# Spreading loads over steps, weight tasks over a longer stretch, and buffers of their own, in a four-stage float32 kernel

## The reference

```python
# 8 batches, 8 heads, 576 tokens, 64 columns a head
kv  = einsum('bhsd,bhse->bhde', k, v)
out = einsum('bhsd,bhde->bhse', q, kv)
x   = out / sqrt(mean(out * out, -1) + 1e-6) * g_norm      # 4608 x 512 tokens
h   = sigmoid(x @ w_gate) * (x @ w_val)                     # 512 -> 1536
y   = h @ w_out                                             # 1536 -> 512
u   = y @ w_in                                              # 512 -> 2048
g   = u where u >= 1, 0 where u <= -1, else (u + 1)**2 / 4
out = g @ w_out2                                            # 2048 -> 512
```

## Time and profile before

| | |
|---|---|
| median of 3 runs | 1786.55 us (1785.83 to 1787.65) |
| profiled execution | 1786.39 us, span 1784.6 us |
| TensorE busy | 1689.6 us, 95% of the span |
| VectorE, ScalarE, GpSimd busy | 68%, 50%, 13% |
| mean granted TensorE clock | 0.974 |
| DMA | 278.90 MB, mean 156 GB/s |

### The profile page before, as it was taken

How to read it: one execution, slowest core, us unless ns; L and a number is a source line. 1 busy time by engine, 2 the same in 40 slices (tenths; PEclk the granted TensorE clock), 3 DMA queues, 4 the chain that set the end, 5 groups by cost and what they waited for, 6 DMA issues and landing times.

```text
span 1784.6 us, 31909 instructions
## 1 busy us (share of the span) xinstructions
PE 1689.6 (95%) x12552; PEld 1651.9 (93%) x12552; DVE 1219.7 (68%) x1723; ACT 888.7 (50%) x1611; POOL 223.5 (13%) x295
## 2 busy tenths in 40 slices
PE   8999999999899999599999889999997899999999
PEld 6789999998899999599999889999997799999999
DVE  4566766676677675477768777777774677667774
ACT  3556666555455544244445455555553444444443
POOL 6210000014443232100001320000001200000000
PEclk9999999999899999899999999999998899999999
DMA  7344434333877779553453333333337954434550
GB/s 256 125 131 138 143 129 136 107 121 117 230 212 206 199 207 276 210 167 126 134 166 138 115 125 131 132 131 132 133 133 248 299 171 136 130 120 128 147 129 36
DMA packets 229316, 278.90 MB, mean 156 GB/s; under 512 B 33072, under 2 KB 172848, under 8 KB 229168
## 3 DMA queue, kind: packets, MB, share of 16 engines
q1 hardware_dynamic: 191568, 207.66, 35.5%
q0 software_dynamic: 37600, 69.22, 13.3%
HBM read 156.76 MB, written 120.06 MB: 155 GB/s over the span
## 4 chain that ended last, share of the span: by engine, by line
PE 64%; DMA 6%; DVE 2%; issue 2%; POOL 2%; SPq 1%; ACT 1%; ACTq 0%; DVEq 0%
PE x L1496 12%; PE x L1498 12%; PE x L1497 12%; PE y L1496 6%; PE y L1498 6%; PE y L1497 6%; DMA fold_lo<-stage 3%; PE z L1496 2%; PE z L1498 2%; PE z L1497 2%; PE h L1496 1%; PE h L1498 1%; PE h L1497 1%; DMA stage<-w_in 1%; DMA g_scratch<-c_tile 1%
## 5 line engine op out<-in xcount | busy, mean ns | idle before, releaser
L1496 PE MATMUL x<-t_hi,v_lo 128*128 128x288 f32 x1664 | 502.6, 302 | 62.9 <-ACT kept L855 19.7
L1497 PE MATMUL x<-t_lo,v_hi 128*128 128x288 f32 x1664 | 496.9, 299 | 0.0
L1498 PE MATMUL x<-t_hi,v_hi 128*128 128x288 f32 x1664 | 495.8, 298 | 0.0
L1496 PEld LDWEIGHTS x<-t_hi,v_lo 128*128 128x128 f32 x1664 | 317.5, 191 | 69.9 <-ACT kept L877 20.5
L1498 PEld LDWEIGHTS x<-t_hi,v_hi 128*128 128x128 f32 x1664 | 319.0, 192 | 0.0
L1497 PEld LDWEIGHTS x<-t_lo,v_hi 128*128 128x128 f32 x1664 | 318.0, 191 | 0.2
L1496 PE MATMUL y<-t_hi,v_lo 128*128 128x288 f32 x832 | 251.5, 302 | 3.3 <-DVE c L1053 1.7
L1497 PE MATMUL y<-t_lo,v_hi 128*128 128x288 f32 x832 | 249.0, 299 | 0.0
L1498 PE MATMUL y<-t_hi,v_hi 128*128 128x288 f32 x832 | 248.2, 298 | 0.0
L1496 PE MATMUL x<-v_hi,t_lo 128*128 128x256 f32 x576 | 164.3, 285 | 6.0 <-ACT o_kept L1018 6.0
L1496 PEld LDWEIGHTS y<-t_hi,v_lo 128*128 128x128 f32 x832 | 159.4, 192 | 7.3 <-DVE c L1053 2.2
(11 more groups left out here) (193 smaller groups left out, 3656.7 us busy)
## 6 DMA issues: line engine op xcount, KB each, us to landing
g_scratch<-c_tile SPq DMA_DIRECT2D x128, 288.0 KB, 2.4
gq<-g_scratch SPq DMA_DIRECT2D x64, 512.0 KB, 6.2
h_scratch<-gate SPq DMA_DIRECT2D x192, 144.0 KB, 2.2
hq<-h_scratch SPq DMA_DIRECT2D x32, 864.0 KB, 5.2
stage<-w_in POOLq DMA_DIRECT2D x68, 256.0 KB, 3.2
kv_ring<-kv_in SPq DMA_DIRECT2D x30, 512.0 KB, 4.5
fold_hi<-fold_hi POOLq DMA_DIRECT2D x14, 896.0 KB, 5.3
fold_lo<-stage POOLq DMA_DIRECT2D x14, 896.0 KB, 7.1
```

What stands on the lines that cost most here:

```text
L1496: nc.tensor.matmul(dst, s_lo, m_hi, start=start, stop=False, skip_group_check=True)
L1497: nc.tensor.matmul(dst, s_hi, m_lo, start=False, stop=False, skip_group_check=True)
L1498: return nc.tensor.matmul(dst, s_hi, m_hi, start=False, stop=stop, skip_group_check=True)
```

## The change

- `SECOND_SETS` and `FOLDS` have new steps; in both, neighbouring tasks stand at least two steps apart.
- GpSimd's loop: sums of t come before the store of fold t-1, and load t+1 after that store has landed. `split_low` is gone; VectorE splits tasks 0 and 1. The sums of tasks 1 and 2 wait for `inv_ready` and `t_ready`.
- VectorE's `split_weights` in stage A moves from the end of a step to before the c12 addition.
- SP reads `hq` one quarter per step in steps 92 to 95, and D's first `gq` quarters one per step in C's last block. B's last three factors and D's last four wait for products of the stage they belong to.
- Stage D's `s_sum` has a place of its own, `gq` of odd units and `o_tile` lie elsewhere; D's first sums and splits stand in C's steps 60 to 64.
- C's tasks 2 to 5 are split earlier in B's last block; the attention of batches 0 and 1 squares into `sq` and its mean is taken chunk by chunk; some roundings and one sum change places.

```diff
-SECOND_SETS = {40: 0, 43: 1, 44: 2, 45: 3, 49: 4, 50: 5}
-FOLDS = {k: i for i, k in enumerate((51, 53, 55, 57, 61, 63, 67, 69, 73, 75, 79, 81, 85, 87))}
+SECOND_SETS = {40: 0, 43: 1, 45: 2, 47: 3, 49: 4, 51: 5}
+FOLDS = {k: i for i, k in enumerate((53, 55, 57, 59, 61, 63, 67, 69, 73, 75, 79, 81, 85, 87))}
...
-              [place(f"gq1{x}", O + (16384 if x == 0 else 41600 + 4096 * (x - 1)), [P, J2, ROWS]) for x in range(4)]]
-        s_sum = place("s_sum", O + 23040, [P, J2, ROWS])
-        o_tile = place("o_tile", O + 27648, [P, 2, 2, DM])
+              [place(f"gq1{x}", O + at, [P, J2, ROWS]) for x, at in enumerate((23040, 27648, 45696, 49792))]]
+        s_sum = place("s_sum", O + 41600, [P, J2, ROWS])
+        o_tile = [place(f"o_tile{i}", O + at, [P, 2, DM]) for i, at in enumerate((16384, 31744))]
...
-                    for x in range(4):
-                        sp.dma_start(hq[x][:], ...).then_inc(hq_loaded[x], 16)
+                if A_STEPS - 4 <= k < A_STEPS:
+                    x = (0, 1, 3, 2)[k - (A_STEPS - 4)]
+                    sp.dma_start(hq[x][:], ...).then_inc(hq_loaded[x], 16)
...
-                    for x in (0, 2, 3, 1):
-                        load_quarter(0, x)
                 for s in range(C_SETS):
+                    if b == C_BLOCKS - 1 and s < 6:
+                        load_quarter(s // 4, (2, 3, 0, 1, 2, 3)[s])
                     store_hidden(C_SETS * b + s)
-            all_stored(sp, g_stored, C_STEPS, 32)
-            for x in (0, 2, 3, 1):
+            for x in range(2):
+                i = (C_STEPS - 3 + x) % 3
+                sp.wait_ge(g_stored[i], 32 * len(range(i, C_STEPS, 3)))
                 load_quarter(1, x)
...
             def load_b(i):
-                if i >= 2:
-                    pool.wait_ge(p_done[3], A_STEPS - A_SETS + min(i - 1, 4))
+                if i == 0:
+                    for parity in range(2):
+                        fold_is_stored(C_TASK - 2 + parity)
+                elif 2 <= i < 4:
+                    pool.wait_ge(p_done[3], A_STEPS - A_SETS + i - 1)
+                elif i >= 4:
+                    pool.wait_ge(p_done[(3, 5, 6)[i - 4]], A_STEPS + min(i - 4, 1))
...
             def load_d(x):
                 pool.wait_ge(p_done[3], D0 - C_SETS + (4 * x + 3) // SEVEN + 1)
+                if x >= 10:
+                    pool.wait_ge(p_done[1 if x < 12 else 5], D0 + 1)
...
-            for task in range(2, TASKS):
+            for task in range(TASKS):
                 pool.wait_ge(stage_loaded[task % 2], 32 * (task // 2 + 1))
+                if task == 1:
+                    pool.wait_ge(inv_ready, 1)
+                elif task == 2:
+                    pool.wait_ge(t_ready, SEVEN)
                 ...                                    # sum_right or sum_left
-                if 3 <= task < TASKS - 1:
-                    if is_fold(task - 1):
+                if is_fold(task - 1):
+                    store_fold(task - 1)
+                    if task == C_TASK:
+                        for i in range(B_LOADS):
+                            load_b(i)
+                    else:
                         fold_is_stored(task - 1)
-                    else:
-                        pool.wait_ge(v_ready, task)
+                elif 0 < task < TASKS - 1:
+                    pool.wait_ge(v_ready, task)
+                if 0 < task < TASKS - 1:
                     load_task(task + 1)
-                if is_fold(task):
-                    store_fold(task)
-                ...
# VectorE, stage A
                 if 1 <= k < 5:
                     split_weights(1 + k)
+                if k in SECOND_SETS:
+                    split_weights(A2_TASK + SECOND_SETS[k])
+                if k in FOLDS:
+                    split_weights(FOLD1_TASK + FOLDS[k])
...                                                    # c12 addition, c11 addition, ...
-                if k in SECOND_SETS: ...
-                if k in FOLDS: ...
+                if k == 0:
+                    split_weights(1)
# ScalarE, B's last block (VectorE alike)
-                        if i == 3:
-                            split_weights(C_TASK + 2)
+                        if 2 <= i < 4:
+                            split_weights(C_TASK + i)
...                                                    # task 4 at i = 5, task 5 at i = 6
# VectorE, C's last steps
-                if k == C_STEPS:
-                    dve.wait_ge(g_stored[(C_STEPS - 3) % 3], 32 * ((C_STEPS - 3) // 3 + 1))
+                if k == C_STEPS - 4:
                     sum_d_item(0, 1)
+                elif k == C_STEPS - 3:
+                    sum_d_item(0, 4)
+                    split_d_item(0, 0)
+                elif k == C_STEPS - 2:
+                    sum_d_item(0, 2)
+                elif k == C_STEPS:
+                    split_d_item(0, 2)
# ScalarE, C
+                if k == 60:
+                    split_d_item(0)
                 if k == C_STEPS - 1:
-                    split_d_item(0)
+                    split_d_item(1)
```

More of the change, by code:

```diff
@@ L521, in store_unit @@
                 for i in range(2):
-                    sp.dma_start(out[tile, first + i, :, :], o_tile[:, u % 2, i, :]).then_inc(out_stored[u % 2], 16)
+                    sp.dma_start(out[tile, first + i, :, :], o_tile[u % 2][:, i, :]).then_inc(out_stored[u % 2], 16)
             all_stored(sp, y_stored, 2 * B_BLOCKS, 32)
@@ L723, in square_heads @@
                 act.wait_ge(head_done, K * n + c + 1)
-                if n < 2:
-                    dst = xo[:, 1 - n, c, :]
-                    if n == 1 and c == 0:
-                        act.wait_ge(t_ready, SEVEN)
-                        for half in range(2):
-                            act.wait_ge(x_stored[half], 16)
+                if n == 0:
+                    dst = xo[:, 1, c, :]
+                elif n == 1:
+                    dst = sq[:]
+                    act.wait_ge(ms_done, K + c)
                 else:
@@ L910, in _ @@
                     scale_heads(1, 3)
-                if s == 2 and b + 1 < B:
-                    split_inverse(b + 1)
                 if heads_of(k + 1):
@@ L1007, in _ @@
                 if k == C_STEPS:
-                    split_d_item(1)
                     split_d_item(2)
+                    split_d_item(3)
                 if k:
@@ L1038, in _ @@
                         reach(act, out_stored[u % 2], 32 * (u // 2))
-                        nc.scalar.copy(o_tile[:, u % 2, 1, 0:R], X[u % 2][:, 0:R]).then_inc(c21_ready, 1)
-                    if u == 0 and j == 0:
-                        split_d_item(4)
+                        nc.scalar.copy(o_tile[u % 2][:, 1, 0:R], X[u % 2][:, 0:R]).then_inc(c21_ready, 1)
                     e = SEVEN * u + j + D_SLOTS
@@ L1269, in _ @@
                     split_query(*heads_of(k))
+                if s == 0 and 0 < b < B:
+                    sum_item(b, 5)
                 if s == 4 and more:
@@ L1314, in _ @@
                     split_square(*heads_of(k))
+                if s == 2 and b + 1 < B:
+                    split_inverse(b + 1)
                 if k:
@@ L1475, in _ @@
                         add(o[:, 0, R:], Y[u % 2][:, 0:R], o_kept[:, 2, :]).then_inc(c12_ready, 1)
-                    if u == 0 and j == 0:
-                        split_d_item(0, 4)
                     nu, i = divmod(SEVEN * u + j + D_SLOTS, SEVEN)
@@ L1543, in first_heads, with first_mean @@
                 last.then_inc(head_done, 1)
-            def first_mean(n):
-                for c in range(K):
-                    pe.wait_ge(sq_raw_ready, K * n + c + 1)
-                    for h in range(2):
-                        last = nc.tensor.matmul(M[0:2 * H, 0:C], head_cols[:, head_window(c, h)],
-                                                xo[:, 1 - n, c, cols(h)], start=c == 0 and h == 0,
-                                                stop=c == K - 1 and h == 1, skip_group_check=True)
-                    last.then_inc(ms_done, 1)
+            def first_mean(n, c):
+                pe.wait_ge(sq_raw_ready, K * n + c + 1)
+                squares = sq[:] if n else xo[:, 1, c, :]
+                for h in range(2):
+                    last = nc.tensor.matmul(M[0:2 * H, 0:C], head_cols[:, head_window(c, h)], squares[:, cols(h)],
+                                            start=c == 0 and h == 0, stop=c == K - 1 and h == 1, skip_group_check=True)
+                last.then_inc(ms_done, 1)
             def heads(n, c):
@@ L1638, in _ @@
                 first_heads(0, c)
-            first_mean(0)
+            for c in range(K):
+                first_mean(0, c)
             kv_chunk(1, 0)
```

88 lines of the change are left out of this document (34 added, 54 removed).

## The result

The changed kernel takes 1760.84 us (median of 4 runs, 1758.69 to 1761.48), the kernel before 1787.1 beside it (4 runs): ratio 0.9851, 95% interval 0.9834 to 0.9868. It is faster by 26 us; forecast were 71, and the range of 1685 to 1750 did not hold it. The profiled execution has a span of 1759.0 us against 1784.6.

What follows compares the result with a forecast made beforehand. TensorE's work plus its gaps and the slow clock behind them was taken as the bound. Terms 10+5+7+21+8+20 = 71 us off 1786.4 gave 1715.4 us; range 1685 to 1750 (8 in 10).

Steps and rivals of the forecast that it cites:

- C to D: Change from stage C to D: 12 us lost instead of 32, gain 20 us (8 to 27).
- The C to D window: Stretch to D's second unit, 97.8 us before; the prediction is wrong if it stays above 90.
- The new wait: C's iteration 60: first D sum waits for the fourth quarter, c12 addition queues behind; TensorE waits 5.5 us plus 1.7.
- Rival 2: C to D: transfers stay the bound, gain 3 us instead of 20, total 1732 (1740 with weaker A to B); chance 0.2.
- Folds: Stage A's weight tasks, steps 40 to 94: 26 us lost instead of 36, gain 10 us.
- The chain: GpSimd's reordered loop in stage A: store, load and sums in series, a period of 16.3 us (15.7 to 18.7).
- The six folds: Stage A, steps 53 to 63, 11.2 us apart: the serial period makes them lose 23.3 us.
- the pairs: Stage A's four later step pairs, 67/69 to 85/87: come out level, at a price of 0.6 us each, 2.4 in all.
- A to B: Change from stage A to B: spread hq reloads and later factor loads leave 2 us lost, gain 21 us (13 to 23).
- B to C: Change from stage B to C: earlier task splits, 5 us lost instead of 13, gain 8 us (3 to 11).
- Start: Kernel start: low parts moved to VectorE and other edits, gain 7 of at most 12 us (low end -2).
- Attention: Stage A's attention: rounding steps moved ahead of a copy or sum, gain 5 us (0 to 7).

Runs made afterwards that it cites:

- e2: Changed kernel with VectorE's first D sums and ScalarE's splits put back to C's steps 63 and 64; 1746.57 us, ratio 0.9759 to the kernel before.
- h1: Changed kernel with only a separate semaphore for the landing of a fold's high part; ratio 0.9824 to the kernel before, steps 40 to 94 in 335.1 us.
- h2: Kernel before with only a separate semaphore for the landing of a fold's high part; ratio 0.9864, steps 40 to 94 in 312.6 us instead of 338.2.
- c2: Changed kernel with the edits of e1, e2 and e4 plus a separate semaphore for a fold's high part; 1717.1 us, ratio 0.9596 to the kernel before.
- e4: Changed kernel with SyncE's first hq reload waiting only for gate stores up to step 53; ratio 0.9823 to the kernel before, step 94 to 95 in 5.6 us.
- e8: Changed kernel with splits of C's weight tasks and first items at the end of B put back as before the change; ratio 0.9855 to the kernel before.
- s1: Changed kernel with VectorE's second low part before the loop of steps; ratio 0.9816 to the kernel before, steps 0 to 2 in 24.1 us instead of 26.3.
- d1: Changed kernel without the loads of the low parts of D's factors (7.3 MB less); ratio 0.9757 to the kernel before, 430.6 us from C's step 56 on.
- e1: Changed kernel with GpSimd's loop in the order of the kernel before (sums, next load, fold store at once); median 1741.96 us, ratio 0.9728.

## Why the prediction was wrong

- **C to D, 20 forecast, -3.7 measured: the step that failed.** Of the 32 us lost here before, 12 were to be left; it became 36, of which TensorE's waits of 18.1 and 8.5 us are 26.6. The C to D window, counted as in the earlier trace rows, is 101 us, and above 90 was named as a sign of a wrong prediction. The new wait was named in its place and its mechanism (the first D sum in iteration 60, the fourth quarter, the c12 addition behind it), and mis-sized: 5.5 us in the text, 18.1 in the trace. The 7.0 us from issue to landing was the median of twelve quarters, eight of them for later units; the one that mattered was issued 7 us late and took 12.8. The kernel before had shown it: the four quarters of unit 0, issued beside such a crowd from 1352.48 on, took 5.9, 8.3, 19.0 and 18.0 us, here the third:

```profile
gq<-g_scratch SPq DMA_DIRECT2D x1, 512.0 KB, 19.0
```

  And the wait was counted once, where unit 1 has it again (8.5). I let the stall "overlap" with the catching up of the transfers. They did go on at 382 GB/s and more for its first 13 us; then the DMA engines fell idle, since GpSimd's next factor load waits for TensorE's products (24.45 us, until 1364.44). The GB/s row of the changed kernel, 1310 to 1400 us in 40 slices, shows 10, 4 and 7 at 1355 to 1362:

```profile
GB/s 164 0 39 223 27 321 275 309 368 379 297 358 398 386 390 385 386 383 382 196 10 4 7 214 295 292 345 241 221 333 398 306 267 103 235 235 310 397 390 382
```

  Rival 2 (the transfers stay the bound, +3) came nearest for this term, but its ground was half of it: e2 wins 15 us with every byte in place.
- **Folds, 10 forecast, 1.8 measured.** The chain was right, 16.3 us forecast and 16.0 to 18.6 measured, and h1 shows that it binds; two sizes were too small. The six folds with the second sets before them lost 29.3 us over pace (40-66) instead of 23.9, the pairs 4.7 instead of 2.4: from the first issue the stores took 8.3 to 11.1 us to land, where I had 8.2 for each, and the products behind a gap run at 1.2 GHz (granted clock 0.50 from 508 to 513 us). Apart from the sum, the reading of the kernel before was wrong: I read "[3.28 <-DMA fold_lo<-stage]" in the earlier trace rows as "the store is late, because the low part is late" and never asked whether the rounding needs fold_lo to land. h2 and c2 show that it doesn't.
- **A to B, 21 and 16.7.** The factor and reload terms held; the SyncE wait for all stores in front of the first reload was not in my sum (e4), nor two waits of TensorE behind the hq sums that stand ahead of two additions (1.1 and 1.6 us, 0.5 and 1.0 in the kernel before).
- **B to C, 8 and 0.9.** The late task was forecast as 8 us per load and sums; they took 8.0, 9.6, 9.9 and 11.1. Single sums last up to 2.5 us instead of 0.73 while VectorE takes a low part of 2.56 us, itself 2.02 when alone. The Trainium skill (SBUF — State Buffer, "Who interferes with whom") has the two engines hold a shared port for a whole instruction, one after the other; the trace agrees with it here, and I had used the page for the start only. That this chain is what held the term down is argued; e8 does not decide it.
- **Start, 7 and 2.3.** s1 shows 2.2 us of it to be one low part behind the item splits, which I had named and not charged.
- **Attention, 5 and 7.6.** Right in kind, and 0.6 us above its own range; steps 2 to 40 take 301.3 to 301.9 us in the profiles with the changed code, 310.4 and 310.8 without it.
- The DMA level held: slices of the crowd reach 398 GB/s, above the 358 GB/s of the Trainium skill (SBUF — State Buffer, "Summary: rules for kernel authors"); with that figure the forecast would have moved by 2 us only.

Five of the six terms came out below the value taken, two below their own range (B to C, C to D). The range I gave each was for one duration; none allowed for a second wait behind the first.

## What to carry to other kernels

A wait for a landing names a buffer: ask which buffer the waiting instruction reuses, and give it the semaphore of that transfer alone; here that one edit, in the kernel before, was worth as much as the whole change. Cost a transfer that an in-order engine will wait for by the slowest row of its kind beside the same crowd, not by a median, and place its consumer as late as its own reader allows. In an in-order loop a store put behind the next task's sums joins landing, load and sums into one period; write that sum down before the order is changed.

## What the hardware showed unasked

Issuing is not free of the crowd. SyncE's two issues of store 58 took 0.80 us with half the factors in flight (d1) and 6.99 and 9.14 us with all of them (the changed kernel, e2), while those of store 57, 5.6 us earlier in the changed kernel, took 0.80; whatever is behind them in the program leaves that much later.

The first k/v chunks do not land at the same time in every execution. Step 0's copy came at 36.1 to 36.9 us in twelve profiles with the changed start (s1 among them) and at 39.5 to 40.2 in three, as here in e1, where TensorE waited for the last chunk and the warming passes behind them took 4.39 us instead of 3.20 (granted clock 0.83 instead of 1.00 from 10 to 20 us). So the span of one execution can't tell 4 us, while its stretches between steps can tell 1. The start term is uncertain by it: where the chunks came early, step 4's copy stands at 82.6 to 85.5 us with the changed start, and at 87.2 and 88.4 in the two profiles with the old one, a gain of 2 to 6 us; in the three late profiles it stands at 88.4 to 88.9, and nothing is left of the gain.

```profile
12.44 1.59 PE L1520 MATMUL m<-xo 64*128 64x128 f32 x8 [0.48 <-DMA xo<-kv_in]
13.96 4.39 PE L1506 MATMUL z<-t_lo 128*128 128x512 bf16 x14
```
